# Queries and keys loaded by head and transposed block by block on VectorE, in a fused attention and two-stage MoE kernel

## The chip, the cores and the metric

The kernel runs on one core of a Trainium2 chip. The metric is the device time of one execution in microseconds (us), as the median of several runs. A core has five instruction streams that run side by side and meet only at semaphores: PE (TensorE, matrix multiply and transpose), DVE (VectorE), ACT (ScalarE), POOL (GpSimd) and SP (SyncE, which here issues every DMA transfer).

## What is computed

Four batches of four heads go through a linear attention whose feature map is the outer product of two 8-wide projections; the result, 4352 tokens of 128 values, goes through a normalised gated layer and then through a soft mixture of 8 experts. Everything is float32.

```python
# q, k, v: (4, 4, 1088, 32), S1, S2: (8, 32)
def phi(x):
    a = np.einsum('rd,bhsd->bhsr', S1, x)
    b = np.einsum('rd,bhsd->bhsr', S2, x)
    return np.einsum('bhsi,bhsj->bhsij', a, b).reshape(*x.shape[:-1], r * r)
q_p, k_p = (phi(q), phi(k))
kv = np.einsum('bhsf,bhsd->bhfd', k_p, v)
z = np.sum(k_p, axis=2)
num = np.einsum('bhsf,bhfd->bhsd', q_p, kv)
den = np.einsum('bhsf,bhf->bhs', q_p, z)[..., None] + 1e-06
attn = num / den
# x = attn as 4352 rows of H * D = 128
rms = np.sqrt(np.mean(x * x, axis=-1, keepdims=True) + 1e-06)
xn = x / rms * rms_g
y = (silu(xn @ w_gate) * (xn @ w_val)) @ w_out      # w_gate, w_val: (128, 1536)
# soft mixture on y: logits = y @ phi (32 slots), softmax over the tokens, the 8 experts
# on their slots (two matrices each), softmax over the slots, and back to the tokens
```

## The kernel before, in words

Each engine's program is written out by hand, in order, and every hand-over is a semaphore with a fixed count. Nothing is scheduled by a tool, so the order in the code is the order on the engine.

A batch has 1088 tokens: eight tiles of 128 tokens (TM = 8) and a remainder of 64 (SR). The queries are worked in nine blocks, two of 512 tokens (HT = 4 tiles) for each batch (blocks 0 to 7) and one of 256 tokens (block 8) with the four remainders.

**The front** prepares the keys and the first query block. It runs over 12 groups G, three for each batch (NG), of three tiles each (G3). SP loads keys, values and queries into tiles that have tokens on the partitions. For batches 0 and 1 DVE brings the keys of a group from the order (head, tile, d) to (tile, head, d) in `k_tok` (L760); for batches 2 and 3 POOL does it in one copy of a whole batch (L376). PE transposes the three tiles (`key_transposes`, L1022), ACT copies the result from PSUM to `kT` (L519), PE projects it (`key_projections`), ACT copies one of the two projections (L525), DVE multiplies the two to the features `kp` (L768), and PE adds features times values up to the moments (`moments`). DVE copies the moments out once for each batch (L750, `head_moments`). Between the groups stand the steps of query block 0: `queries_by_token` (DVE L619), `queries_T` (PE L882, ACT L437), `projections`, `features` (DVE L628, L630), `features_T` (PE L902, ACT L445), `attention` (PE, then DVE L640 to L650), `squares` (ACT L451), `mean_square` (DVE L657), the inverse root on POOL (L382), `normalised` (DVE L666), `normalised_T` (PE L925, ACT L455) and `split_x` (DVE L672, L674). The three weight matrices of the gated layer are split in a high and a low part on the way: ACT writes the high parts (L506), POOL the low ones (`wgl` L379, `wvl` L384, `wol` L386), in its order wgl, inverse root of block 0, wvl, wol.

**The blocks.** `whole_block` runs over 12 chunks c of 128 hidden columns. In each chunk PE does three matmuls for the gate, three for the value (`gate_value`) and three for the output of three chunks earlier (`output`); ACT takes silu of the gate (L476) and the high part of the hidden values (L484), DVE multiplies gate and value (L695) and forms the low part (L701). The attention of block j + 1 is spread over block j: in the kernel before, `queries_T` at c = 0, `projections` at c = 1, `features_T` at c = 2, `attention` at c = 4, `normalised_T` at c = 7. Every fp32 matmul and transpose is one row in the trace that ends at a line of a helper: L859 is the matmul helper.

**The end** computes the softmaxes and the experts, and SP stores the tokens.

## Time and profile before

| | before |
|---|---|
| median of 3 runs | 333.32 us (331.68 to 333.97) |
| span of the profiled execution | 332.9 us |
| PE busy | 304.8 us (92%) |
| DVE busy | 226.0 us (68%) |
| ACT busy | 176.2 us (53%) |
| POOL busy | 33.3 us (10%) |
| share of PE in the chain that ended last | 83% |

The profiled execution is 0.4 us shorter than the median of the runs; all start times below are counted from its own start. The span falls in three stretches: the front from 0 to 46.7 us, when the first matmul of block 0 starts; the nine blocks from there to about 300 us; and the end. A line of the timeline gives an operation's start, its length, engine and line of the kernel, what it writes and reads, how many instructions it groups, and in square brackets how long the engine had been idle before it and whose signal ended that. "area" is one of the large shared buffers, "bank" is PSUM. The chain of waits is read backwards from the last instruction and names what each piece waited for last.

### The profile page before, as it was taken

The page shows a single profiled execution, that of the slowest core. Times are in us where ns is not written, and L with a number is a line of the kernel's source. Part 1 is how long each engine was busy: PE and PEld are TensorE (multiplying, and loading weights), DVE is VectorE, ACT ScalarE, POOL GpSimd, SP SyncE. Part 2 cuts the span into 40 slices and gives each one's busy share as a digit, 9 for nine tenths or more (in the row PEclk, how much of TensorE's full clock was granted, in tenths as well). Part 3 has the DMA queues.
Part 4 walks back from the last instruction along what each step waited for, and adds up shares of the span by engine and source line. Part 5 has one row for each costly group of instructions (what it writes and reads, how often), then busy time and mean ns, then how long its engine had stood idle before and what let it go on. Part 6 is the DMA issues. An engine that isn't in the chain of part 4 may idle for free.

```text
span 332.9 us, 6852 instructions
## 1 busy us (share of the span) xinstructions
PE 304.8 (92%) x2596; PEld 245.2 (74%) x2596; DVE 226.0 (68%) x442; ACT 176.2 (53%) x333; POOL 33.3 (10%) x51
## 2 busy tenths in 40 slices
PE   1997539999999999999999999999999999997993
PEld 1786437878888878878888787888878778895472
DVE  4657765686858667775866777676677667974364
ACT  2657206555556654665665465566645656555410
POOL 1116470010001001100100110010001001001000
PEclk9999778999999999999999999999999999999997
DMA  6995019100100000059500000000000000000008
GB/s 185 301 346 139 3 36 417 53 0 2 63 2 1 0 3 2 0 156 290 121 0 0 0 0 0 0 0 0 0 0 1 0 2 0 3 0 3 2 22 248
DMA packets 25654, 19.97 MB, mean 60 GB/s; under 512 B 4129, under 2 KB 24353, under 8 KB 25633
## 3 DMA queue, kind: packets, MB, share of 16 engines
q1 hardware_dynamic: 25632, 19.68, 20.1%
q8 instruction: 14, 0.23, 0.3%
q14 instruction: 8, 0.06, 0.1%
HBM read 17.45 MB, written 2.23 MB: 59 GB/s over the span
## 4 chain that ended last, share of the span: by engine, by line
PE 83%; DVE 9%; ACT 3%; issue 2%; DMA 1%; SPq 0%; POOL 0%; DVEq 0%; ACTq 0%
PE bank L859 74%; PE bank L902 2%; DVE y_nat L850 2%; PE bank L1022 2%; DVE xh L672 2%; PE bank L945 1%; DVE area L666 1%; PE bank L925 1%; DMA area<-in_k 1%; PE bank L882 1%; DVE hl L701 1%; PE bank L1128 1%; DVE hid L695 1%; ACT woh L506 0%; DVE ssq L657 0%
## 5 line engine op out<-in xcount | busy, mean ns | idle before, releaser
L695 DVE TENSOR_TENSOR hid<-bank,silu 128x512 f32<-128x512 f32 (+1 forms) x108 | 71.3, 661 | 72.8 <-PE bank L859 58.9
L476 ACT ACTIVATE silu<-bank 128x512 f32<-128x512 f32 (+1 forms) x108 | 61.8, 572 | 81.7 <-PE bank L859 80.1
L701 DVE TENSOR_TENSOR hl<-hid,hh 128x512 fp32r<-128x512 f32 (+1 forms) x108 | 70.6, 654 | 0.1
L484 ACT ACTIVATE hh<-hid 128x512 fp32r<-128x512 f32 (+1 forms) x108 | 64.7, 599 | 0.9 <-PE bank L859 0.7
L859 PE MATMUL bank<-xh,wgh 128*128 128x512 f32 (+1 forms) x117 | 47.8, 408 | 6.2 <-DVE xl L674 5.9
L859 PE MATMUL bank<-xh,wgl 128*128 128x512 f32 (+1 forms) x117 | 44.9, 384 | 0.0
L859 PE MATMUL bank<-xl,wgh 128*128 128x512 f32 (+1 forms) x117 | 44.9, 384 | 0.0
L859 PE MATMUL bank<-hh,woh 128*128 128x512 f32 (+1 forms) x108 | 43.8, 405 | 0.4 <-DVE hl L701 0.4
L859 PE MATMUL bank<-xh,wvl 128*128 128x512 f32 (+1 forms) x108 | 41.6, 385 | 0.0
L859 PE MATMUL bank<-xh,wvh 128*128 128x512 f32 (+1 forms) x108 | 41.5, 385 | 0.0
L859 PE MATMUL bank<-xl,wvh 128*128 128x512 f32 (+1 forms) x108 | 41.2, 382 | 0.0
L859 PE MATMUL bank<-hh,wol 128*128 128x512 f32 (+1 forms) x108 | 41.1, 380 | 0.0
L859 PE MATMUL bank<-hl,woh 128*128 128x512 f32 (+1 forms) x108 | 40.9, 378 | 0.0
L859 PEld LDWEIGHTS bank<-xh,wgh 128*128 128x128 f32 x117 | 22.4, 192 | 10.5 <-issue 6.0
L401 POOL TENSOR_TENSOR rstd<-msq,mhalf 128x4 f32<-128x4 f32 (+1 forms) x8 | 7.8, 970 | 189.2 <-DVE msq L659 189.2
L859 PEld LDWEIGHTS bank<-xh,wgl 128*128 128x128 f32 x117 | 22.4, 191 | 4.6
L859 PEld LDWEIGHTS bank<-xl,wgh 128*128 128x128 f32 x117 | 22.5, 192 | 3.6
L859 PEld LDWEIGHTS bank<-xl,wvh 128*128 128x128 f32 x108 | 20.6, 190 | 4.2
L859 PEld LDWEIGHTS bank<-xh,wvl 128*128 128x128 f32 x108 | 20.6, 190 | 4.2
L859 PEld LDWEIGHTS bank<-hh,woh 128*128 128x128 f32 x108 | 20.3, 188 | 4.6 <-DVE hl L701 0.6
L859 PEld LDWEIGHTS bank<-xh,wvh 128*128 128x128 f32 x108 | 20.6, 190 | 4.0
L859 PEld LDWEIGHTS bank<-hh,wol 128*128 128x128 f32 x108 | 20.3, 188 | 4.1
(151 smaller groups left out, 372.4 us busy)
## 6 DMA issues: line engine op xcount, KB each, us to landing
area<-in_moe_w SPq DMA_DIRECT2D x1, 4096.0 KB, 12.7
area<-in_moe_w SPq DMA_DIRECT2D x8, 512.0 KB, 7.3
area<-in_k SPq DMA_DIRECT2D x4, 512.0 KB, 6.2
y_nat<-in_v SPq DMA_DIRECT2D x4, 512.0 KB, 6.4
q_in<-in_q SPq DMA_DIRECT2D x4, 512.0 KB, 4.3
out<-y_nat SPq DMA_DIRECT2D x8, 256.0 KB, 2.9
area<-in_moe_w_gate SPq DMA_DIRECT2D x1, 768.0 KB, 8.2
area<-in_moe_w_val SPq DMA_DIRECT2D x1, 768.0 KB, 8.8
```

The costliest lines, as they stand in the source:

```text
L401: pool.tensor_tensor(rstd[:, 0:nt], msq[:, 0:nt], mhalf[:, 0:nt], ALU.pow).then_inc(s_rstd_ready, 1)
L476: act.activation(silu[n][:, 0:w], gate_b[n][:, 0:w], ACT.Silu).then_inc(s_silu_ready, 1)
L484: act.activation(hh[m % NH][:, 0:w], hid[m % 2][:, 0:w], ACT.Copy).then_inc(s_hh_ready, 1)
L666: dve.tensor_tensor(x_n[:, 0:nt, :], x_at[:, 0:nt, :], rstd[:, 0:nt].unsqueeze(2).to_broadcast([P, nt, P]), ALU.mult).then_inc(s_xn_ready, 1)
L672: dve.tensor_copy(xh[n][:, 0:w], xT_raw[:, 0:w]).then_inc(s_xh_ready, 1)
L695: dve.tensor_tensor(hid[n][:, 0:w], val_b[n][:, 0:w], silu[n][:, 0:w], ALU.mult).then_inc(s_hid_ready, 1)
L701: dve.tensor_tensor(hl[m % NH][:, 0:w], hid[m % 2][:, 0:w], hh[m % NH][:, 0:w].bitcast(F32), ALU.subtract).then_inc(s_hl_ready, 1)
L850: dve.tensor_tensor(o_sb[:, HT * j:HT * j + nt, :], bank[2 + n % 6][:, 0:nt * P].rearrange("p (t d) -> p t d", d=P), crec[:, HT * j:HT * j ...
L859: return pe.matmul(o, l, r, start=start, stop=stop)
L882: ins = pe.transpose(bank_a[:, t * P:(t + 1) * P], tile, ident[:, :])
L902: ins = pe.transpose((bank_a, bank_c)[hp][:, t * P:(t + 1) * P], qp[:, t, hp * P:(hp + 1) * P], ident[:, :])
L1022: ins = pe.transpose(kT_b[:, t * P:(t + 1) * P], k_tok[G // NG % 2][:, G3 * (G % NG) + t, :, :].rearrange("p h d -> p (h d)"), ident[:, :])
```

## The change

Queries and keys are loaded with the 32 partitions of a head holding 32 runs of consecutive tokens of that head (`"h (u n) d -> h u (n d)"`), so that a key transfer of 8 tiles has one run of 4 KB for each of the 128 partitions, where it had four of 1 KB; the remainder has one run of 256 B on 128 partitions, where it had four of 128 B on 64. The queries are loaded by half batch, with one run of 2 KB on each partition and a semaphore for each half. DVE then transposes 32x32 blocks straight from the loaded tile to `kT` and `qT`. This is the transposed layout that the projections read, since head h occupies the 32 partitions from 32h on both sides. The values' tile (partition p holds tokens 8p to 8p + 7) and the tokens of a key tile stay matched. The tokens of a query block are now 512 consecutive ones, and the store of the output follows that.

What falls away: on PE the 36 key transposes and the 34 query transposes; on ACT the 12 copies to `kT` and the 9 to `qT`; on DVE the six copies L760 and the four L619; on POOL the two copies L376. What comes: on DVE one transpose for each key group (4 x 96 columns, or 4 x 64 and another of 2 x 32 for the third group of a batch) and one for each query block (4 x 128 columns; 256 for block 8). `kT` now holds a whole batch, twice, so that DVE runs four groups ahead: groups 0 to 3 stand ahead of the loop, group G + 4 behind the features of group G.

Of the diff, the loads, ACT's copy to `kT`, the two new functions of DVE and their calls in the front, the wait that `features_T` takes over on PE, and the store (in this order):

```diff
-        k_in = [area1[:, n * KW:(n + 1) * KW].rearrange("p (h t d) -> p h t d", h=H, t=TK) for n in range(B)]
-        k_tok = [area1[:, (B + n) * KW:(B + n + 1) * KW].rearrange("p (t h d) -> p t h d", h=H, t=TK) for n in range(2)]
-        kT = [area1[:, (B + 2) * KW + n * G3 * P:(B + 2) * KW + (n + 1) * G3 * P] for n in range(2)]
+        KB_MAIN, KB_REM = TM * P // D, SR // D
+        KC = (KB_MAIN + KB_REM) * D
+        k_in = [area1[:, n * KC:(n + 1) * KC] for n in range(B)]
+        kT = [area1[:, B * KC + n * TK * P:B * KC + (n + 1) * TK * P] for n in range(2)]
...
-        q_in = sb("q_in", [P, H, TM, D])
-        q_rem = sb("q_rem", [P, 2, H, D])
-        q_tok = sb("q_tok", [P, TM, H * D])
+        q_in = sb("q_in", [P, 2, W])
+        q_rem = sb("q_rem", [P, B, SR // D, D])
...
+            def load_queries(b, half):
+                sp.dma_start(q_in[:, half, :],
+                             q[b, :, half * W:(half + 1) * W, :].rearrange("h (u k) d -> h u (k d)", u=D))\
+                    .then_inc(s_q_loaded[half], 16)
+
             for b in range(B):
-                for src, dst, loaded in ((k, k_in[b], k_loaded[b]), (v, v_in[b], v_loaded[b])):
-                    sp.dma_start(dst[:, :, 0:TM, :],
-                                 src[b, :, 0:TM * P, :].rearrange("h (p t) d -> p h t d", t=TM)).then_inc(loaded, 16)
-                    sp.dma_start(dst[0:SR, :, TM, :],
-                                 src[b, :, TM * P:S, :].rearrange("h p d -> p h d")).then_inc(loaded, 16)
+                sp.dma_start(k_in[b][:, 0:KB_MAIN * D],
+                             k[b, :, 0:TM * P, :].rearrange("h (u n) d -> h u (n d)", u=D)).then_inc(k_loaded[b], 16)
+                sp.dma_start(k_in[b][:, KB_MAIN * D:KC],
+                             k[b, :, TM * P:S, :].rearrange("h (u n) d -> h u (n d)", u=D)).then_inc(k_loaded[b], 16)
...
+            sp.wait_ge(s_qT_ready, 1)
+            load_queries(1, 0)
             sp.wait_ge(s_kv_ready, B)
             sp.dma_start(w1_sb, w1.rearrange("e d f -> d e f")).then_inc(s_w1_loaded, 16)
+            for n in range(3, 2 * B):
+                sp.wait_ge(s_qT_ready, n - 1)
+                load_queries(n // 2, n % 2)
...
-                if G < B * NG:
-                    act.wait_ge(s_kT_ps, G + 1)
-                    if later(G - 1):
-                        act.wait_ge(s_kab_ps, G - 1)
-                    act.activation(kT[G % 2], kT_b[:, 0:G3 * P], ACT.Copy).then_inc(s_kT_ready, 1)
...
+            def queries_T(jn, half, b):
+                if isinstance(jn, int) and jn == NB:
+                    dve.wait_ge(s_qrem_loaded, 16 * B)
+                    src = q_rem[:, :, :, :]
+                    dst = qT[:, 0:B * SR].rearrange("p (b u r) -> p b r u", b=B, r=SR // D)
+                else:
+                    dve.wait_ge(s_q_loaded[half], b * 16 + 16)
+                    src = q_in[:, half, :].rearrange("p (i t d) -> p i t d", i=P // D, t=HT)
+                    dst = qT.rearrange("p (t u i) -> p i t u", t=HT, i=P // D)
+                if later(jn):
+                    dve.wait_ge(s_ab_ps, jn)
+                dve.transpose(dst, src).then_inc(s_qT_ready, 1)
+
+            def keys_T(G):
+                b, g = G // NG, G % NG
+                if g == 0:
+                    dve.wait_ge(k_loaded[b], 32)
+                if later(G + 1 - 2 * NG):
+                    dve.wait_ge(s_kab_ps, G + 1 - 2 * NG)
+                t0, t1 = G3 * g, min(G3 * g + G3, TM)
+                src = k_in[b][:, 0:KB_MAIN * D].rearrange("p (i t d) -> p i t d", i=P // D, t=TM)
+                dst = kT[b % 2][:, 0:TM * P].rearrange("p (t u i) -> p i t u", t=TM, i=P // D)
+                ins = dve.transpose(dst[:, :, t0:t1, :], src[:, :, t0:t1, :])
+                if g == NG - 1:
+                    ins = dve.transpose(kT[b % 2][:, TM * P:TM * P + SR].rearrange("p (u r) -> p r u", r=KB_REM),
+                                        k_in[b][:, KB_MAIN * D:KC].rearrange("p (r d) -> p r d", r=KB_REM))
+                ins.then_inc(s_kT_ready, 1)
...
+            for G in range(4):
+                keys_T(G)
             for G in range(B * NG):
...
                 if G % NG == 1 and G > NG:
                     head_moments(G // NG - 1)
+                if G + 4 < B * NG:
+                    keys_T(G + 4)
                 if G == 2:
-                    queries_by_token(0, 0)
+                    queries_T(0, 0, 0)
...
+                if later(jn):
+                    pe.wait_ge(s_xT_ready, jn)
...
-                    rows = out[b * S:b * S + TM * P, :].rearrange("(p t) d -> p t d", t=TM)
-                    sp.dma_start(rows[:, t0:t0 + HT, :], o_sb[:, j * HT:(j + 1) * HT, :]).then_inc(s_out_stored, 16)
+                    rows = out[b * S + t0 * P:b * S + (t0 + HT) * P, :].rearrange("(p t) d -> p t d", t=HT)
+                    sp.dma_start(rows, o_sb[:, j * HT:(j + 1) * HT, :]).then_inc(s_out_stored, 16)
```

The first place is PE inside the blocks, at the change from chunk c = 0 to c = 1. Before, these are the rows there; `hh` and `wo` belong to `output`, `xh` and `w` to `gate_value`, and `q_tok` is the query tile in token order.

```order
L859 MATMUL bank<-hh,woh 128x512 [waits hl_ready]
L859 MATMUL bank<-hl,woh 128x512
L859 MATMUL bank<-hh,wol 128x512
L877 REGISTER_ALU
L882 MATMUL bank<-ident,q_tok 128x128 [waits xT_ready,qtok_ready]
L882 MATMUL bank<-ident,q_tok 128x128 x3
L962 REGISTER_ALU
L859 MATMUL bank<-xh,wgh 128x512 [waits hid_ready]
```

And now, where L858 is the matmul helper of the changed kernel:

```order
L858 MATMUL bank<-hh,wol 128x512
L950 REGISTER_ALU
L858 MATMUL bank<-xh,wgh 128x512 [waits hid_ready]
L858 MATMUL bank<-xl,wgh 128x512
L858 MATMUL bank<-xh,wgl 128x512
L858 MATMUL bank<-xh,wvh 128x512
L858 MATMUL bank<-xl,wvh 128x512
L858 MATMUL bank<-xh,wvl 128x512
L872 REGISTER_ALU
L874 REGISTER_ALU [waits qT_ready]
```

The four transposes have gone from between the output of one chunk and the gate of the next; the projections one chunk later still wait for `qT_ready`, which is now DVE's signal and not ACT's.

The second place is DVE in the front, from the features of group 0 on. Before (L768 features of a key group, L619 queries to token order):

```order
L760 COPY area<-area 128x384 [waits k_loaded1]
L760 COPY area<-area 128x384 x2
L768 TENSOR_TENSOR area<-bank,logit 128x768 [waits kb_ready]
L768 TENSOR_TENSOR comb<-bank,logit 128x768 [waits kb_ready]
L768 TENSOR_TENSOR logit<-bank,logit 128x768 [waits kb_ready]
L619 COPY q_tok<-q_in 128x1024 [waits q_loaded]
L768 TENSOR_TENSOR area<-bank,logit 128x768 [waits kb_ready,kmom_done]
L768 TENSOR_TENSOR comb<-bank,logit 128x768 [waits kb_ready,kmom_done]
```

And now (L618 and L620 transpose keys, L607 queries, L765 is the features' line):

```order
L618 STREAM_TRANSPOSE area<-area 128x4x96 [waits k_loaded1]
L765 TENSOR_TENSOR area<-bank,logit 128x768 [waits kb_ready]
L618 STREAM_TRANSPOSE area<-area 128x4x96
L765 TENSOR_TENSOR comb<-bank,logit 128x768 [waits kb_ready]
L618 STREAM_TRANSPOSE area<-area 128x4x64
L620 STREAM_TRANSPOSE area<-area 128x2x32
L765 TENSOR_TENSOR logit<-bank,logit 128x768 [waits kb_ready]
L618 STREAM_TRANSPOSE area<-area 128x4x96 [waits kab_ps,k_loaded2]
L607 STREAM_TRANSPOSE area<-q_in 128x4x128 [waits q_loaded0]
L765 TENSOR_TENSOR area<-bank,logit 128x768 [waits kb_ready,kmom_done]
L618 STREAM_TRANSPOSE area<-area 128x4x96 [waits kab_ps]
```

Three copies in a row behind the arrival of batch 1 have become one transpose, and behind every group's features up to group 7 stands another one; the keys of batches 2 and 3, which POOL had, are now in DVE's row too.

## Rows read from the trace of the kernel before

**Rows 1.** The page, its head and part 1: busy time of each engine.
```profile
span 332.9 us, 6852 instructions
PE 304.8 (92%) x2596; PEld 245.2 (74%) x2596; DVE 226.0 (68%) x442; ACT 176.2 (53%) x333; POOL 33.3 (10%) x51
```
**Rows 2.** Busy time by window: length, then busy us of each engine, clock, DMA.
```profile
74.33:103.96 29.63, 29.63 (x209) 23.95 (x209) 20.65 (x37) 16.86 (x30) 1.01 (x1) 1.00 0.06 19
103.96:133.59 29.63, 29.63 (x210) 23.96 (x209) 20.80 (x39) 17.37 (x32) 1.41 (x2) 1.00 0.01 2
10.19:30.34 20.15, 18.36 (x387) 15.62 (x386) 14.42 (x29) 12.98 (x28) 5.75 (x3) 1.00 1.01 293
```
**Rows 3.** The chain that ended last, one block: start, length, what.
```profile
103.96 10.99 PE bank L859 x48
114.95 0.44 PE bank L882 x4
115.39 4.97 PE bank L859 x34
```
**Rows 4.** Query transposes on PE, grouped by form.
```profile
L882 PE MATMUL bank<-ident,q_tok 128*128 128x128 f32 x32 | 4.8, 273 | 0.0
```
**Rows 5.** What PE waited for, whole span: us, times, longest.
```profile
PE bank L859 <- DVE xl L674: 5.9, 1, 5.9
PE bank L925 <- DVE area L666: 4.3, 2, 3.8
```
**Rows 6.** Timeline of DVE in the front.
```profile
10.19 1.47 DVE L760 COPY area<-area 128x384 f32<-128x384 f32 x3 [2.78 <-DMA area<-in_k]
26.14 0.96 DVE L768 TENSOR_TENSOR comb<-bank,logit 128x768 f32<-128x768 f32 x1 [3.14 <-ACT logit L525]
...
28.11 0.25 DVE L643 RECIPROCAL rden<-den 128x16 f32<-128x16 f32 x1
...
30.34 0.69 DVE L657 TENSOR_REDUCE ssq<-area 128x4 f32<-128x512 f32 x1 [0.32 <-ACT area L451]
...
32.36 3.90 DVE L666 TENSOR_TENSOR area<-area,rstd 128x512 f32<-128x512 f32 x1 [0.27 <-POOL rstd L382]
...
40.64 5.22 DVE L672 CAST xh<-area 128x512 fp32r<-128x512 f32 x1 [1.01 <-ACT area L455]
```
**Rows 7.** Timeline of POOL in the front.
```profile
15.65 1.15 POOL L376 COPY area<-area 128x1152 f32<-128x1152 f32 x1 [13.30 <-DMA area<-in_k]
19.36 1.15 POOL L376 COPY area<-area 128x1152 f32<-128x1152 f32 x1 [2.56 <-DMA area<-in_k]
...
26.86 3.46 POOL L379 TENSOR_TENSOR wgl<-area,wgh 128x1536 fp32r<-128x1536 f32 x1 [6.35 <-ACT wgh L506]
31.30 1.02 POOL L382 TENSOR_TENSOR rstd<-msq,mhalf 128x4 f32<-128x4 f32 x1 [0.99 <-DVE msq L659]
32.30 3.42 POOL L384 TENSOR_TENSOR wvl<-area,wvh 128x1536 fp32r<-128x1536 f32 x1
```
**Rows 8.** Timeline of ACT in the front.
```profile
23.70 0.84 ACT L506 ACTIVATE wgh<-area 128x768 fp32r<-128x768 f32 x1 [2.14 <-DMA area<-in_moe_w_gate]
...
30.70 0.85 ACT L506 ACTIVATE wvh<-area 128x768 fp32r<-128x768 f32 x1
```
**Rows 9.** DVE instructions that price a transpose, grouped by form: busy us, mean ns.
```profile
L657 DVE TENSOR_REDUCE ssq<-area 128x4 f32<-128x512 f32 x8 | 5.4, 679 | 0.3 <-ACT area L451 0.3
L760 DVE COPY area<-area 128x384 f32<-128x384 f32 x6 | 2.9, 546 | 4.6 <-DMA area<-in_k 4.6
L619 DVE COPY q_tok<-q_in 128x1024 f32<-128x1024 f32 x4 | 2.7, 685 | 0.0
L724 DVE TENSOR_REDUCE cmax_a<-logit 128x32 f32<-128x896 f32 x1 | 1.8, 1792 | 0.0
L836 DVE TENSOR_REDUCE csum<-comb 128x34 f32<-128x1088 f32 x1 | 1.3, 1276 | 0.0
L797 DVE TENSOR_REDUCE cmax<-logit 128x32 f32<-128x192 f32 x1 | 0.5, 502 | 0.0
```
**Rows 10.** DMA packets in the windows 6 to 10 us and 52 to 58 us.
```profile
DMA packets 1697, 1.21 MB, mean 303 GB/s; under 512 B 576, under 2 KB 1697, under 8 KB 1697
DMA packets 609, 2.49 MB, mean 416 GB/s; under 512 B 0, under 2 KB 0, under 8 KB 609
```
**Rows 11.** Timeline of DVE in a block, around c = 0.
```profile
114.37 0.69 DVE L695 TENSOR_TENSOR hid<-bank,silu 128x512 f32<-128x512 f32 x1 [0.77 <-PE bank L859]
114.98 0.68 DVE L701 TENSOR_TENSOR hl<-hid,hh 128x512 fp32r<-128x512 f32 x1
116.89 0.69 DVE L695 TENSOR_TENSOR hid<-bank,silu 128x512 f32<-128x512 f32 x1 [1.23 <-PE bank L859]
```

More of the change, by code:

```diff
@@ L170, in fused_attention_moe @@
         s_wo_loaded = sem("wo_loaded")
-        s_q_loaded = sem("q_loaded")
+        s_q_loaded = [sem(f"q_loaded{n}") for n in range(2)]
         s_qrem_loaded = sem("qrem_loaded")
@@ L370, in _ @@
             pool.memset(kv[:, :, :, :], 0.0).then_inc(s_kvpads_ready, 1)
-            pool.wait_ge(s_kpads_ready, B)
-            for b in range(2, B):
-                pool.wait_ge(k_loaded[b], 32)
-                pool.wait_ge(s_kT_ps, (b - 1) * NG)
-                pool.tensor_copy(k_tok[b % 2], k_in[b].rearrange("p h t d -> p t h d")).then_inc(s_ktok23_ready, 1)
             pool.wait_ge(s_wg_hi, 2)
@@ L492, in whole_block @@
                     step(j, c)
-                    if c == 0 and not last:
-                        queries_T(j + 1)
                     if c == 2 and not last:
@@ L591, in _ @@
         def _(dve):
-            for n in range(B):
-                dve.memset(k_in[n][SR:P, :, TM, :], 0.0).then_inc(s_kpads_ready, 1)
+            for n in range(2):
+                dve.memset(kT[n][:, TM * P + SR:TK * P], 0.0).then_inc(s_kTpads_ready, 1)
             for n in range(B):
@@ L706, in whole_block @@
                 for c in range(-LAG if first else 0, C):
-                    if c == 0 and odd and nb is not None:
-                        queries_by_token(j + 1, nb)
+                    if c == 0 and not last:
+                        queries_T(j + 1, odd ^ 1, nb)
                     step(j, c)
@@ L752, in head_moments @@
                 ins.then_inc(s_kv_ready, 1)
-            dve.wait_ge(s_kpads_ready, B)
-            for b in range(2):
-                dve.wait_ge(k_loaded[b], 32)
-                for g in range(NG):
-                    tiles = slice(g * G3, (g + 1) * G3)
-                    dve.tensor_copy(k_tok[b][:, tiles], k_in[b].rearrange("p h t d -> p t h d")[:, tiles])\
-                        .then_inc(s_ktok01_ready, 1)
+            for G in range(4):
+                keys_T(G)
             for G in range(B * NG):
@@ L783, in _ @@
             head_moments(B - 1)
-            whole_block(0, 0, first=True)
+            whole_block(0, 0, 0, first=True)
             with dve.Fori(1, B) as b:
@@ L869, in _ @@
             pe.wait_ge(s_sblk_ready, H)
-            def queries_T(jn, half, b):
-                if isinstance(jn, int) and jn == NB:
-                    pe.wait_ge(s_qrem_loaded, 16 * B)
-                    tiles = [q_rem[:, n, :, :].rearrange("p h d -> p (h d)") for n in range(2)]
-                else:
-                    pe.wait_ge(s_qtok_ready, b + 1)
-                    tiles = [q_tok[:, HT * half + t, :] for t in range(HT)]
-                if later(jn):
-                    pe.wait_ge(s_xT_ready, jn)
-                for t, tile in enumerate(tiles):
-                    ins = pe.transpose(bank_a[:, t * P:(t + 1) * P], tile, ident[:, :])
-                ins.then_inc(s_qT_ps, 1)
             def projections(jn):
```

66 lines of the change are left out of this document (16 added, 50 removed).

## The prediction

> **What bounds the kernel now.** The page comes first: PE is busy for 304.8 of 332.9 us, DVE for 226.0 [rows 1]. Such shares are means over stages, so the windows come next. A whole block takes 29.63 us, and in it PE is busy for 29.63 us, DVE for 20.7 (twice the same to 0.2 us) [rows 2]. The chain of waits of a block is made of PE alone; what is taken off PE there comes off the time, and DVE has 8.9 us to spare. One piece of that chain is the query transposes, 0.44 us [rows 3].
>
> The front is another matter. The table of PE's waits has 5.9 us in front of the first matmul of block 0 and 4.3 for L666 [rows 5]. The timelines show why. DVE's L666 takes 3.90 us, where L657 on as many elements takes 0.69, and it starts 0.06 us after POOL's wvl of 3.42 us; L672 takes 5.22 us behind wol in the same way [rows 6, 7]. So from L657 at 30.34 on, the front is one chain: mean square, inverse root to 32.32, wvl and L666 to 36.3, the last two groups, wol and L672, first matmul at 46.7. It starts later or earlier as L657 does. Ahead of L657 DVE had to wait: of 20.15 us from the arrival of key batch 1 to L657 it is busy for 14.42, so idle for 5.7 [rows 2]. The longest wait, 3.14 us ahead of 26.14, is for ACT, which itself waited for w_gate until 23.70 and so copied features_T late [rows 6, 8].
>
> **Blocks: query transposes leave PE.** They are issued 8 times with four tiles, once in the front and for blocks 1 to 7 [rows 4], and with two for block 8. In the chain of a block the four cost 0.44 us. 7 x 0.44 = 3.1, and half of 0.44 for block 8: **-3.3 us**. All other PE work stays. DVE loses L619 of 685 ns every second block and gets a transpose of 512 columns in every block. Whatever this costs between 0.68 and 1.09 us (below), it stands at c = 0 ahead of L695, where DVE sits idle for 0.77 us waiting for PE in the chunks around [rows 11]; what is over delays L695 by 0.3 us at most, and idle time of the same size stands ahead of the next one. DVE's total goes to some 21.5 of 29.2 us. Projections wait one chunk later, 2 us on. If that cover were gone, PE would wait with L695 and the whole 1.09 us would show eight times, once in each block from 0 to 7. ACT's 0.6 us copy was off the chain: nothing. The queries' loads are issued a block or two ahead and w2's after them, over 100 us before their use: nothing. The store has as many runs of 512 B as before: nothing.
>
> **Front: what the transfers give.** From 6 to 10 us the loads run at 303 GB/s in runs of 1 KB and below; w1 with runs of 4 KB runs at 416 [rows 10]. 524 KB of a key batch then take 1.26 instead of 1.73 us, 0.45 less, and the remainder half as many packets. The arrival of batch 1 (10.19) moves up by two of these, 1.0 us with the smaller remainder, to 9.2; w_gate has four of them (1.8) and the queries in 2 KB runs (estimated 0.3) ahead of it, so it is there at 21.6. Bounds: nothing, and these.
>
> **Front: what DVE gets.** No row shows a transpose on DVE, nor a write with a step. Lower bound, one element per cycle: L760 has 546 ns for 384 elements and L657 679 for 512; L657 and L836 make 1.04 ns for one more element and 0.15 us at the start. Upper bound: L724 and L797 read with each element 128 bytes on, 1792 ns for 896 and 502 for 192, so 1.83 ns each [rows 9]. The transpose writes with a step of 16 bytes. From L657 back to the arrival of batch 1 there are six transposes of 384, three of 256 with one of 64, and one of 512:
> - low price: 6 x 0.55 + 3 x (0.41 + 0.21) + 0.68 = 5.8 us
> - high price: 6 x 0.85 + 3 x (0.62 + 0.27) + 1.09 = 8.9 us
>
> Off go three L760 (1.47, rows 6) and L619 (0.68): 14.42 - 2.15 = 12.3 us stay. At the high price DVE is busy for 21.2 us from 9.2 on; that fills its former idle time, and some 0.4 us of waits remain: L657 at 30.8, **+0.4 us**. At the low price it is 18.1 us and about 1.3 of waits (features_T through PE and ACT stay on the way to group 7): 28.6, -1.7 us. I take the high price: the write's step puts no two elements next to each other, and of the rows only L724 and L797 do that. **A wait moves to DVE.** The keys of batches 2 and 3, which POOL fetched at 15.65 and 19.36 [rows 7], are now waited for by DVE itself, and behind that instruction stand the query transpose, the features of group 3 and all that follows. DVE comes there after three features (2.9 us) and three groups of transposes: at the high price 9.2 + 2.9 + 2.6 = 14.7, at the low one 13.8, against an arrival at some 14.1 (three key batches and the queries earlier by 1.6). So 0.3 us at the low price, nothing at the high one; batch 3 is in by 17.5, before DVE is through group 5.
>
> ACT's twelve copies and PE's key transposes were hidden beside DVE and w_gate and give nothing by themselves; what PE no longer does only shortens the way from kT to kb. Behind L657 all stays: the high part of w_val (ready at 31.55, inverse root at 32.32 [rows 7, 8]) is still first, so wvl still catches L666.
>
> The notes speak against this edit: the Trainium skill, "SBUF — State Buffer", on the port swizzle (its box on cachelines), says that each access which moves on to another 16-byte line pays a penalty; by that the high price holds, +0.4 us here, and the reads of L724 and L797 agree, while no row shows it for a write.
>
> **Sum.** 332.9 - 3.3 + 0.4 = 330.0 us of span; the median of the runs is 0.4 above the profiled execution, so **330.4 us** (329.8 to 331.4, the upper end with none of the transfers' gain: batch 1 at 10.2 gives L657 at 31.8).
>
> **Rivals.**
> - *Transposes at the low price.* For it speaks that DVE's contiguous copies and reductions keep to a cycle each, and writes need not behave like reads. -3.3 - 1.7: 328.3 us (327.7 to 330.0, the upper end with w_gate as late as before and group 7 again behind it). Chance 0.33. The Trainium skill, "VectorE: DVE Perf Modes", section "The three transpose paths", has 311 ns for 128x128 in bf16; an estimate from this page's figure is the low price and this time. No row here has a transpose on DVE to hold against it.
> - *DVE's transposes are held up by POOL like L666.* wgl (3.46 us) follows the high part of w_gate and would lie on the keys of group 10 or 11: +2.5 us on the forecast, 332.9. Against it: L666 and L672 read SBUF through what POOL uses, but L643, one input in SBUF, took 0.25 us in the middle of wgl's 3.46 and so was not held up [rows 6, 7]. Chance 0.05.
> - *A transpose of 4-byte data takes several passes.* This is the rival on the other side. 6 x 384 + 3 x 320 + 512 = 3776 elements lie ahead of L657, and thirteen starts of 0.15 us, 1.95 us. To lose 1% (3.3 us) over no change the front must give 6.6 us more, L657 at 37.0 instead of 30.3: 27.8 us of work from 9.2 on, of which 12.3 stay, 13.5 go to the elements: 3.6 ns each, twice the high price. At four cycles (4.2 ns) it is +8.9 - 3.3, 338.9 us. Between 1.83 and 3.6 ns it ends within 1%. Chance 0.07 beyond 3.6, 0.08 between 2.3 and 3.6 (332 to 336.6).
> - *The inverse root gets in ahead of wvl.* If the high part of w_val came over 0.8 us later, L666 would run in 0.7 and save 3.2 us: 327.2. ACT has less to do, so this moves away. 0.02.
>
> **How the numbers follow.** Forecast 0.45, low price 0.33, POOL 0.05, dearer 0.08 and 0.07, inverse root 0.02. About 1% is what a measurement of this kernel can tell from no change, 330.0 us downwards and 336.7 upwards. Faster: 0.33 + 0.02 and a third of the forecast's 0.45, since 330.4 stands so near 330.0: 0.50. Slower: 0.07. Same: 0.43. The range 327.6 to 333.6 takes in both prices with and without the transfers' gain and POOL's hold, and leaves out the dearer transposes and the inverse root, 0.17.
>
> **What would show it.** Right: blocks of 29.2 us, with PE busy throughout and no new wait on DVE L697 or qT; keys' transposes of 0.85 us for 384 columns; key batch 1 in by 9.2 and w_gate by 21.6 us; no wait of DVE above 1 us between groups 3 and 8; first matmul of block 0 at about 47.1 us. Wrong: 0.55 us per transpose, first matmul at 45; or a transpose far above 1 us, with PE and ACT idle in the front; or a block of 29.6, which would mean that the transposes had been hidden on PE after all.

## The result and the profile after

| | before | after |
|---|---|---|
| median of the runs (range) | 333.64 us (331.68 to 334.18) | 353.72 us (352.26 to 354.22) |
| span of the profiled execution | 332.9 us | 351.4 us |
| first matmul of block 0 | 46.73 us | 69.45 us |
| a whole block | 29.63 us | 29.17 us |
| key batch 1 / w_gate in use | 10.19 / 23.70 us | 20.10 / 45.86 us |

The change makes the kernel slower: ratio 1.0594, interval 1.0551 to 1.0637. The first matmul of block 0 comes 22.7 us later, and what follows it takes 281.95 us instead of 286.17, 4.2 us less. The blocks gave what was forecast, and the front lost five times as much.

The page of the kernel after: busy time, then the granted clock, the share of the 16 DMA engines that is busy and what they move, in 40 slices of 8.8 us.

```profile
PE 299.0 (85%) x2526; PEld 243.1 (69%) x2526; DVE 235.8 (67%) x455; ACT 166.0 (47%) x312; POOL 31.3 (9%) x49
...
PE   0141583499999999999999999999999999998993
...
PEclk9996567689999999999999999999999999999999
DMA  4444840084000000000000794000000000000008
GB/s 89 134 137 133 246 132 17 2 343 167 0 0 32 0 3 30 2 1 4 26 0 0 138 271 98 0 0 0 0 0 0 2 0 3 0 2 2 0 8 248
```

PE is fully at work from the ninth slice on; up to then it mostly waits, and the DMA engines are busy for four tenths at 89 to 137 GB/s (in the fifth slice for eight tenths, at 246), where the front before had 303 [rows 10]. The waits of the kernel after, over the whole span (waiting engine and line, who ends the wait, total, times, longest):

```profile
POOL wgl L373 <- ACT wgh L494: 46.3, 1, 46.3
...
DVE area L618 <- DMA area<-in_k: 25.0, 4, 8.2
...
ACT area L516 <- DMA y_nat<-in_v: 11.6, 1, 11.6
```

DVE waited for keys four times, 25.0 us. The chain of waits goes through the last key batch: the second of its two loads is issued at 29.97 us, and the batch is there 12.45 us later.

```profile
29.97 12.45 DMA area<-in_k
```

In DVE's timeline these waits stand in brackets, and the rest of the front follows (start, length, line):

```profile
12.10 2.01 DVE L618 STREAM_TRANSPOSE area<-area 128x384 f32<-128x384 f32 x3 [8.12 <-DMA area<-in_k]
...
20.10 0.85 DVE L618 STREAM_TRANSPOSE area<-area 128x384 f32<-128x384 f32 x1 [5.93 <-DMA area<-in_k]
...
33.10 0.85 DVE L618 STREAM_TRANSPOSE area<-area 128x384 f32<-128x384 f32 x1 [8.16 <-DMA area<-in_k]
33.80 1.05 DVE L607 STREAM_TRANSPOSE area<-q_in 128x512 f32<-128x512 f32 x1
...
42.45 0.86 DVE L618 STREAM_TRANSPOSE area<-area 128x384 f32<-128x384 f32 x1 [2.83 <-DMA area<-in_k]
...
53.29 0.69 DVE L659 TENSOR_REDUCE ssq<-area 128x4 f32<-128x512 f32 x1 [0.60 <-ACT area L441]
...
55.31 3.90 DVE L668 TENSOR_TENSOR area<-area,rstd 128x512 f32<-128x512 f32 x1 [0.27 <-POOL rstd L376]
...
63.59 4.98 DVE L674 CAST xh<-area 128x512 fp32r<-128x512 f32 x1 [1.01 <-ACT area L445]
```

Key batch 3 is in use at 42.45 us, where POOL had it at 19.36 [rows 7], 23.1 us late; the mean square (L659, before L657 at 30.34 [rows 6]) starts 22.95 us late. Behind it all is as it was, 3.90 us beside wvl included. A whole block, by windows (length, busy us of PE, PEld, DVE, ACT, POOL, clock, DMA share, GB/s), against [rows 2]:

```profile
95.82:125.00 29.18, 29.18 (x205) 23.56 (x205) 20.92 (x37) 16.28 (x29) 1.01 (x1) 1.00 0.03 10
125.00:154.17 29.17, 29.17 (x206) 23.57 (x205) 21.64 (x40) 16.80 (x31) 1.41 (x2) 1.00 0.03 10
```

And DVE's transposes by form (busy us, mean ns):

```profile
L607 DVE STREAM_TRANSPOSE area<-q_in 128x512 f32<-128x512 f32 x8 | 8.8, 1100 | 0.0
...
L618 DVE STREAM_TRANSPOSE area<-area 128x384 f32<-128x384 f32 x8 | 6.7, 856 | 25.0 <-DMA area<-in_k 25.0
...
L618 DVE STREAM_TRANSPOSE area<-area 128x256 f32<-128x256 f32 x4 | 2.6, 642 | 0.1
...
L607 DVE STREAM_TRANSPOSE area<-q_rem 128x256 f32<-128x256 f32 x1 | 0.4, 439 | 0.0
```

The last two lines have 256 columns each, and only the first of them costs the high price. It writes with a step of 16 bytes; the transpose of the query remainders (`q_rem`, two tokens of a head to a partition) writes with a step of 8 bytes.

So blocks, transposes and order came out as forecast, and the transfers did not. What slows them? Theory A: the number of engines that carry a DMA load is the largest one, up to 16, that divides the sizes of the outermost parts of both its patterns. The keys' source now begins with the 4 heads, so each load of keys and queries runs on 4 engines; before, it began with 128 token groups. The Trainium skill, "DMA: Bandwidth & Descriptors", section "Why a DMA increments its semaphore by 16 and not by 1", states this rule, with the lowest-numbered engines taken, so that such loads also share the same ones. The trace agrees: from 10 to 12 us, where key batch 1 is under way with the end of the values, the engines' share is 0.28. Rivals: DVE's new place in the chain (it now waits for the keys itself), or something in the loads' size, number or order of addresses.

### The profile page after: what moved, and what is told of

Its sections match the earlier page's. It is cut to its first block, busy times and chain, and to the rows that moved or that the text cites. A ratio compares the mean times of both kernels' runs of the same rounds, so it can differ in the third digit from the quotient of the medians.

```text
span 351.4 us, 6670 instructions
## 1 busy us (share of the span) xinstructions
PE 299.0 (85%) x2526; PEld 243.1 (69%) x2526; DVE 235.8 (67%) x455; ACT 166.0 (47%) x312; POOL 31.3 (9%) x49
## 4 chain that ended last, share of the span: by engine, by line
PE 75%; DVE 8%; SPq 8%; DMA 4%; ACT 2%; issue 1%; POOL 0%; DVEq 0%; ACTq 0%
PE bank L858 68%; SPq L316 4%; DMA area<-in_k 4%; PE bank L890 2%; SPq L312 2%; DVE y_nat L849 2%; DVE xh L674 1%; PE bank L933 1%; DVE area L668 1%; PE bank L913 1%; SPq L310 1%; DVE hl L703 1%; PE bank L1100 1%; DVE hid L697 1%; SPq L305 1%
## 5 line engine op out<-in xcount | busy, mean ns | idle before, releaser
L858 PE MATMUL bank<-xh,wgh 128*128 128x512 f32 (+1 forms) x117 | 46.9, 400 | 5.3 <-DVE xl L676 5.0
L858 PE MATMUL bank<-xh,wgl 128*128 128x512 f32 (+1 forms) x117 | 45.0, 384 | 0.0
L858 PE MATMUL bank<-xl,wgh 128*128 128x512 f32 (+1 forms) x117 | 44.6, 382 | 0.0
L858 PE MATMUL bank<-hh,woh 128*128 128x512 f32 (+1 forms) x108 | 43.8, 405 | 0.4 <-DVE hl L703 0.4
L858 PE MATMUL bank<-xh,wvh 128*128 128x512 f32 (+1 forms) x108 | 41.4, 384 | 0.0
L858 PE MATMUL bank<-xh,wvl 128*128 128x512 f32 (+1 forms) x108 | 41.4, 383 | 0.0
L858 PE MATMUL bank<-hh,wol 128*128 128x512 f32 (+1 forms) x108 | 41.1, 380 | 0.0
L858 PE MATMUL bank<-xl,wvh 128*128 128x512 f32 (+1 forms) x108 | 41.0, 380 | 0.0
L858 PE MATMUL bank<-hl,woh 128*128 128x512 f32 (+1 forms) x108 | 40.9, 379 | 0.0
L858 PE MATMUL bank<-s_blk,area 128*64 128x64 f32 x280 | 15.2, 264 | 25.6 <-DVE area L618 10.0
L858 PEld LDWEIGHTS bank<-s_blk,area 128*64 128x64 f32 x280 | 12.7, 171 | 29.6 <-issue 21.4
L858 PEld LDWEIGHTS bank<-xh,wgh 128*128 128x128 f32 x117 | 22.3, 190 | 9.7 <-issue 5.1
L618 DVE STREAM_TRANSPOSE area<-area 128x384 f32<-128x384 f32 (+1 forms) x12 | 9.1, 785 | 25.1 <-DMA area<-in_k 25.0
L858 PEld LDWEIGHTS bank<-xh,wgl 128*128 128x128 f32 x117 | 22.3, 190 | 4.5
L858 PEld LDWEIGHTS bank<-xl,wgh 128*128 128x128 f32 x117 | 22.4, 191 | 3.9
L858 PEld LDWEIGHTS bank<-xl,wvh 128*128 128x128 f32 x108 | 20.6, 190 | 4.2
L858 PEld LDWEIGHTS bank<-hh,woh 128*128 128x128 f32 x108 | 20.3, 188 | 4.6 <-DVE hl L703 0.6
```

Source lines behind the costliest of these rows:

```text
L618: ins = dve.transpose(dst[:, :, t0:t1, :], src[:, :, t0:t1, :])
L858: return pe.matmul(o, l, r, start=start, stop=stop)
```

## The experiments

**The loads alone, in the kernel before.** Key loads as in the change, all else as before:

```diff
-  sp.dma_start(k_in[b][:, :, 0:TM, :], k[b, :, 0:TM*P, :].rearrange("h (p t) d -> p h t d", t=TM))
+  sp.dma_start(k_flat[:, 0:TM*P],      k[b, :, 0:TM*P, :].rearrange("h (u n) d -> h u (n d)", u=D))
```

> The kernel before with one part of the change alone: the keys (main part and remainder) are loaded in the changed form, head by head with 32 runs of 4 KB each; all else is as before, so keys and values no longer match by token and the output differs. Theory A (the key and query loads whose source pattern starts with the 4 heads run on a quarter of the DMA engines: in the changed kernel's trace the DMA share stands at 0.2 to 0.3 and 98 GB/s while they run, some 5.2 us for 524 KB): key batches arrive at about 12, 20, 28 and 37 us, w_gate after 40, first matmul of block 0 near 63, time near 350 us, DMA share near a quarter for long stretches. Theory B (DVE's transposes or the new order of the front are the cause): 333 to 335 us, since neither is in this kernel.

354.46 us, ratio 1.0614 (1.0575 to 1.0653): as slow as the whole change, with PE and ACT still transposing keys and queries. DVE's first two key copies waited 8.22 and 7.27 us for keys, w_gate was used at 41.94, and the first matmul of block 0 came at 66.53, a little after the 63 expected. The loss is there without anything that DVE does in the change. (The two kernels are not the same sum: this one has neither the blocks' gain nor the slow query loads.)

**The other way round.** The kernel after, with the main key loads, and then the query loads too, in the form of before (same bytes and work, other places):

> The changed kernel with the main part of the keys loaded in the old form (128 partitions first, four runs of 1 KB each); the key remainder, the queries, the transposes and the order stay as changed. The transposes then work on keys in another token order, so the output differs, not the work. Theory A: the keys cost 1.7 us each again, only the two loads for query block 0 and 1 are still slow (5.2 us together, 3.6 more than before) and push batches 2 and 3 and w_gate back; first matmul near 52 us, time 334 us. Theory B: no change from the changed kernel, 353 us. Theory C (the remainder's small runs of 256 B stop the queue, on whose issue SP stands for up to 7.5 us): no change either, 350 to 353 us.

> As the run before, and the queries' loads too in a form with 128 partitions first (runs of 512 B); token order and so output differ. This leaves of the change what DVE, PE, ACT and POOL do. Theory A: arrivals as in the kernel before, first matmul at 48 to 49 us (the transposes at 0.85 us for 384 columns, as priced), blocks of 29.2 us: 330 to 331 us. Theories B and C: near 350 us.

Keys alone: 337.68 us, 1.0085 (1.0057 to 1.0112). Keys and queries: 332.31 us, 0.9946 (0.9923 to 0.9969), key batches used at 6.13, 10.23 and 16.02 us, w_gate at 23.38, first matmul at 47.80. The keys' loads carry 16 us of the loss and the queries' 5.4. Both kernels are slower than was expected for them: 337.68 against 334 (first matmul 53.12 against 52), and 332.31 against 330 to 331, part of it because the kernel before took 334.04 beside them and not 333.32. DVE of the second kernel, its key waits and the mean square:

```profile
6.13 2.02 DVE L618 STREAM_TRANSPOSE area<-area 128x384 f32<-128x384 f32 x3 [2.16 <-DMA area<-in_k]
...
10.23 0.86 DVE L618 STREAM_TRANSPOSE area<-area 128x384 f32<-128x384 f32 x1 [2.02 <-DMA area<-in_k]
...
31.42 0.67 DVE L659 TENSOR_REDUCE ssq<-area 128x4 f32<-128x512 f32 x1
```

**Cut into four, cut into two.** The same runs and addresses as after, as one load per head (keys and queries), and as one load per two heads (keys):

```diff
-  sp.dma_start(k_in[b][:, 0:1024], k[b, :, 0:1024, :].rearrange("h (u n) d -> h u (n d)", u=D))
+  for h in range(H):        # e4
+      sp.dma_start(k_in[b][h*D:(h+1)*D, 0:1024], k[b, h, 0:1024, :].rearrange("(u n) d -> u (n d)", u=D))
+  for x in range(2):        # e8
+      sp.dma_start(k_in[b][x*64:(x+1)*64, 0:1024], k[b, 2*x:2*x+2, 0:1024, :].rearrange("h (u n) d -> h u (n d)", u=D))
```

> The changed kernel, whole, with the same runs from the same addresses to the same places, but each key and query load issued as four, one for each head, so that 32 runs and not 4 heads come first in each. Theory A: every piece is spread over all engines; key batch 1 in by 9 to 10 us, w_gate by 22 to 25 (SP has 17 more issues of about 0.5 us), first matmul at 47 to 50 us, time 329 to 332 us. Theory D (runs of 4 KB from this layout are slow in themselves, by their length or addresses): still 350 us. Theory C: still near 350 us, since the remainder is unchanged.

> The kernel after, with each of the four main key loads cut into two, one for two heads each; same bytes, runs and addresses, nothing left out. Theory A (the outermost part of a load's pattern sets how many of the 16 engines carry it, and always the first ones): a load for two heads is carried by two engines, and both halves by the same two, so the cut makes it worse. The first two engines then carry 2.1 MB of keys between them, in the kernel after four did; with the other loads that is 1.5 MB to an engine instead of 1.0 MB, and at the 25 GB/s per engine of the kernel after (about 100 GB/s on four) the last weight comes some 20 us later: 370 to 378 us. Rival B (each load has its own engines or its own rate, so more loads run side by side, as the cut into four loads gained 18 us): between the kernel after (353.7 us) and the cut into four (335.4 us), about 345 us.

One load of four heads 353.72 us, two loads 373.54 (ratio 1.1186, from two runs), four loads 335.39 (1.0040). Cutting once makes it 20 us worse, cutting again 38 us better, of which the queries, cut only in the second kernel, can hold some 5 (above). An effect of the loads' size, number or addresses alone would not turn round like this, and theory A had the 373.5 in its 370 to 378. The windows show the engines counted out. First the kernel after, then the one with head pairs, both where hardly anything but keys is under way:

```profile
10.00:12.00 2.00, 0.00 (x0) 0.00 (x0) 0.00 (x0) 0.00 (x0) 0.00 (x0) 1.00 0.28 84
```

```profile
10.00:12.00 2.00, 0.00 (x0) 0.00 (x0) 0.00 (x0) 0.00 (x0) 0.00 (x0) 1.00 0.13 51
12.00:14.00 2.00, 0.00 (x0) 0.00 (x0) 0.00 (x0) 0.00 (x0) 0.00 (x0) 1.00 0.13 51
14.00:16.00 2.00, 0.00 (x0) 0.00 (x0) 0.00 (x0) 0.00 (x0) 0.00 (x0) 1.00 0.13 49
```

0.13 of 16 is 2 engines, 0.28 is 4 and a little. 51 GB/s over two is 25 GB/s each, about what 416 GB/s over 16 make [rows 10]; in the kernel after it is 19 GB/s each in this window. So with pairs each engine runs near its full rate, and there are too few of them.

By-head loads do not get all of it back: 335.39 us where 329 to 332 were expected, key batch 1 at 11.12 us and w_gate at 28.33. The number of loads is part of it: SP issues w_gate at 21.12 us, where before it did so at 15.48. But the DMA engines were not idle either. These are the windows from 6 to 14 us of the kernel before and of this one (the last two columns are the DMA share and GB/s; the share adds up the time of the packets, so it can pass 1):

```profile
6.00:14.00 8.00, 6.08 (x72) 4.53 (x72) 5.02 (x9) 4.10 (x9) 0.00 (x0) 1.00 1.12 310
```

```profile
6.00:14.00 8.00, 2.43 (x40) 2.30 (x42) 4.88 (x8) 1.55 (x3) 0.00 (x0) 1.00 1.04 250
```

At nearly the same share they moved a fifth less. Each of these loads goes to 32 partitions only; e9 and e10 below show the same with values.

**Keys of a whole batch in one load.** 34 tokens of one head to a partition are one run of 4352 B, and 128 of them the whole batch:

```diff
-  k[b, :, 0:1024, :].rearrange("h (u n) d -> h u (n d)", u=D)      # and one for the remainder
+  k[b].rearrange("h (u n) d -> (h u) (n d)", u=D)                  # e5; e6: "h (u n) d -> h u (n d)"
-  dst = kT[...].rearrange("p (t u i) -> p i t u", ...)
+  dst = kT[...].rearrange("p (t i u) -> p i t u", ...)             # dense writes
```

> The kernel after, with the loads of the front in a form whose outermost part is long, so that on theory A they are spread over 16 engines: a key batch is one load of 128 rows of 4352 B (34 tokens of one head to a partition, remainder included), the values follow in six loads of 32 partitions (same tokens, 1 KB and 128 B runs), the first 512 queries in four loads by head, the second 512 behind the weights. The key transposes also write densely now (each 32 outputs side by side), while the query transpose still writes with its 16-byte step. All work is done, nothing is left out. Theory A (few engines per load were the whole loss): key batch 1 in by 9, no wait of VectorE above 2 us in the front, w_gate in by 23, blocks of 29.17 us, and a time below the kernel before. On the price of the transposes: if the 16-byte step of the write is what made them 0.85 us for 384 columns, they take 0.55 us now beside 1.09 us for the 512 queries, the mean square starts at about 29 us, and the time is 328.5 to 329.5 us; if it is the transpose itself, they stay at 0.85 us, the mean square starts at 30 to 31 us and the time is 330 us. Rival (the transfers are slow because of short runs or the number of bytes): batch 1 after 12 us, time above 335 us.

> e5 with one thing changed: the source of each key load is written as 4 heads x 32 rows x 4352 B in place of 128 rows x 4352 B. Same bytes, same addresses, same 128 runs, same number of loads. Theory A in its strict form (the outermost part as written decides how many engines a load gets): key batches come as late as in the kernel after (batch 1 after 12 us, w_gate after 30 us), time 345 to 352 us. If neighbouring dimensions are merged before the engines are chosen, there is no difference to e5. Rival (something in the order of addresses): also no difference to e5, since the addresses are the same.

e5 333.86 us (0.9995, 0.9966 to 1.0024), e6 334.62 (1.0009, 0.9974 to 1.0043): no difference between them. With 34 of 34 tokens the heads follow each other without a gap, so 4 x 32 rows are 128 rows, and the way it is written does not matter. In the change, 1024 of 1088 tokens leave a gap between heads, and the 4 stays outermost. Theory A in its strict form (345 to 352 us expected for e6) is ruled out; it holds for the pattern after such merging.

e5 missed its 328.5 to 329.5 us, though. The price part came true: the dense key transposes take 565 ns for 384 columns, while the query transpose, still with the 16-byte step, keeps its price in the same kernel:

```profile
L621 DVE STREAM_TRANSPOSE area<-area 128x384 f32<-128x384 f32 x8 | 4.4, 565 | 7.7 <-DMA area<-in_k 7.7
...
L610 DVE STREAM_TRANSPOSE area<-q_in 128x512 f32<-128x512 f32 x1 | 1.1, 1056 | 0.0
```

But DVE still waited 7.7 us for keys. Two kernels took this apart: values loaded in two loads as before (e9), and by head to all 128 partitions (e10).

> e5 with the values loaded as in the kernel before, in two loads of 128 and 64 partitions for a batch instead of six of 32 partitions. The rows of values then belong to other tokens than the keys they are paired with; the work is the same. In e5 the 16 engines were busy all the time from 6 to 18 us and yet moved only 241 GB/s, against 316 in the query-part-alone kernel. If the value loads of 32 partitions are what is slow: above 290 GB/s from 6 to 14 us, key batch 1 in by 9.5 instead of 11.35 us, batch 2 by 14 instead of 17.4, w_gate by 23, and 329 to 330 us. If it is the key load with rows of 4352 B: rates and arrivals as in e5, 333 to 334 us.

> e5 with the main part of the values in four loads by head, each to all 128 partitions, instead of four by groups of 32 partitions; the key transposes write with their 16-byte step again, since the tokens of a partition are others. Nothing is left out. If a load to 32 partitions is what is slow, the transfers are those of e9: key batch 1 by 9.5 us, w_gate by 23 us; VectorE has 0.28 us more for each key transpose, 2 us in all before the mean square, of which the waits that fall away give back as much: 330 to 331 us. If the number of loads is what is slow (SyncE issues 32 of them at 0.46 us before w_gate), w_gate is as late as in e5 and the time is 334 to 335 us.

The window 6 to 14 us of e5, e9 and e10, in this order (last two columns: DMA share, GB/s):

```profile
6.00:14.00 8.00, 2.46 (x41) 2.33 (x43) 3.84 (x8) 1.56 (x3) 0.00 (x0) 1.00 1.10 244
```

```profile
6.00:14.00 8.00, 3.96 (x69) 3.83 (x70) 5.02 (x11) 2.86 (x5) 0.00 (x0) 1.00 1.06 322
```

```profile
6.00:14.00 8.00, 3.49 (x60) 3.36 (x62) 5.20 (x11) 2.55 (x5) 0.00 (x0) 1.00 0.74 223
```

e9: 329.58 us, 0.9864 (0.9825 to 0.9904), within its forecast; key batch 1 used at 9.87 us, w_gate at 21.50, first matmul at 45.33. (It pairs keys with values of other tokens, so it shows a time and is no kernel to use.) e9 also has fewer loads than e5; e10, with as many as e5, separates the two. For each full share of the 16 engines e5 moved 222 GB/s (244 over 1.10), e9 304 and e10 301. So the value loads of 32 partitions are what slowed e5: all engines busy, each a quarter slower. The Trainium skill, "SBUF — State Buffer", section "Door 1: The DMA port swizzle", has a transfer's rate go by the SBUF ports that its partitions reach; 244 against 322 GB/s agrees in direction, and no run here gives a rate for such loads by themselves. e10: 333.43 us, 0.9989 (0.9955 to 1.0024), not the 330 to 331 expected: key batch 1 at 10.07 us, but the engines only 0.74 busy and w_gate not before 25.48. For w_gate SP is the limit: four value loads take it 2.5 us to issue, 0.62 us each, in every batch, and it issues w_gate at 20.65 us, where e9 does so at 11.51:

```profile
12.13 2.48 SPq L312 DMA_DIRECT2D y_nat<-in_v  x4
```

Both causes exist, one in each kernel, and I had not expected the second to remain. It is the smaller part, though. The mean square starts 3.3 us later than in e9: DVE is busy 2.0 us longer from key batch 1 on (19.55 against 17.53 us), since its transposes cost 865 ns again with the 16-byte step, and it waits 1.0 us more for ACT, which waits for w_gate.

**The query half alone.** The kernel before, with queries transposed by DVE and keys untouched (the first 512 queries in four loads by head):

> The kernel before with the query half of the change alone: queries transposed by VectorE, no PE transposes and ScalarE copies of queries; keys and values are loaded and transposed as before. The first 512 queries come in four loads by head, the second 512 behind the weights. If the gain of the change sits wholly in the blocks: 8 blocks 0.46 us shorter, -3.7 us, and in the front the query transpose of 1.09 us takes the place of a copy of 0.68 us, +0.4 us: 3.3 us under the kernel before, 330.5 us, blocks of 29.17 us, first matmul of block 0 within 0.7 us of 46.7. If the keys' half also carries some of the block gain, the blocks stay above 29.17 us.

330.53 us, 0.9901 (0.9863 to 0.9939), as expected for the time. Blocks of 29.17 us: the chain of this kernel has L856 after the transposes at 98.35 and the same at 127.52.

```profile
97.91 0.44 PE bank L911 x4
98.35 15.94 PE bank L856 x82
...
127.09 0.44 PE bank L911 x4
127.52 2.52 PE bank L856 x11
```

All the block gain is the query half's. The profiled execution was the quickest of the eight (326.78 us): the first matmul came at 43.30 us, not within 0.7 of 46.7, and 2.05 us of that are the high part of x, which took 3.17 us in it instead of 5.22. It ended at 42.43, with POOL's product wol (to 42.14); in the kernel before it ended at 45.86, after POOL's memset behind wol (to 45.35). What the slower executions do is not traced.

**POOL beside DVE.** The length of these instructions beside POOL's led to two kernels that let POOL's products wait until DVE is through:

```diff
+  pool.wait_ge(s_xn_ready, 1)     # e11 and e12, ahead of wvl
   pool.wait_ge(s_wv_hi, 2)
...
+  pool.wait_ge(s_xl_ready, 1)     # e12, ahead of wol
   pool.wait_ge(s_wo_hi, 2)
```

> The query-part-alone kernel with one more wait: POOL computes the low part of w_val (wvl) behind VectorE's normalisation of block 0 (the instruction that takes 3.90 us beside wvl, 0.7 us alone on as many elements) instead of just ahead of it. Nothing is left out. If wvl beside it is what makes it 3.90 us: it takes 0.7 us, all that follows moves up by 3.2 us, wvl is done by 36 us and still in time for its first matmul; 327.3 us. The low part of w_out still lies on the high part of x (5.2 us). If its length has another cause: 3.90 us as before, and 330.5 us or, with wvl later, up to 331.

> The kernel of e11 with a second wait of the same kind: the low part of w_out (wol) behind VectorE's high and low part of x. If wol beside it is what makes the high part 5.22 us, it takes 0.7 us and the first matmul of block 0 comes 4.5 us earlier still, at about 38 us; 322.8 to 324 us. If PE then waits in block 0 for wol, up to 1 us of that is lost. If the length has another cause: as e11.

e11: 326.77 us, 0.9784 (0.9755 to 0.9813). e12: 319.66 us, 0.9573 (0.9545 to 0.9602), the quickest kernel here, 4.3% under the one before. DVE and POOL of e12 (before: 3.90 and 5.22 us for the two [rows 6]):

```profile
32.20 0.69 DVE L665 TENSOR_TENSOR area<-area,rstd 128x512 f32<-128x512 f32 x1 [0.27 <-POOL rstd L382]
...
36.48 0.43 DVE L671 CAST xh<-area 128x512 fp32r<-128x512 f32 x1 [1.01 <-ACT area L452]
```

```profile
32.97 3.46 POOL L385 TENSOR_TENSOR wvl<-area,wvh 128x1536 fp32r<-128x1536 f32 x1 [0.81 <-DVE area L665]
...
37.71 3.53 POOL L388 TENSOR_TENSOR wol<-area,woh 128x1536 fp32r<-128x1536 f32 x1 [1.28 <-DVE xl L673]
```

With nothing of POOL beside it the normalisation takes 0.69 us and the cast 0.43. In e11, where wvl ends at 36.4 and wol follows at once, the cast took 5.66 us, past wol and past POOL's memset behind it. The Trainium skill, "SBUF — State Buffer", section "Who interferes with whom", says that a port pair shared by VectorE and GpSimd is locked for a whole instruction; these rows agree for both forms. e12 gained 7.1 us over e11, where 4.5 at most were expected for the cast. The rest is TensorE's clock. PE in e11 and then e12, its first matmuls of block 0 and, below, the window from there on:

```profile
42.95 0.77 PE L857 MATMUL bank<-xh,wgh 128*128 128x512 f32 x1 [6.11 <-DVE xl L672]
43.52 0.63 PE L857 MATMUL bank<-xl,wgh 128*128 128x512 f32 x1
```

```profile
42.95:55.00 12.05, 12.04 (x59) 9.57 (x60) 8.54 (x15) 5.62 (x11) 1.47 (x6) 0.87 0.86 335
```

```profile
37.77 0.47 PE L858 MATMUL bank<-xh,wgh 128*128 128x512 f32 x1 [0.87 <-DVE xl L673]
38.08 0.40 PE L858 MATMUL bank<-xl,wgh 128*128 128x512 f32 x1
```

```profile
37.77:50.00 12.23, 12.22 (x70) 9.96 (x71) 9.94 (x17) 6.55 (x12) 8.40 (x12) 1.00 0.88 335
```

e12's 322.8 to 324 us was missed by 3 us on the good side. After a wait of 6.1 us PE starts at 0.63 us a matmul, and the mean clock of the next 12 us is 0.87 (the lower of the two levels, 1.2 GHz, for a part of it); after a wait of 0.87 us it starts at 0.40, at 2.4 GHz throughout. 13% of 12 us is 1.6 us. Of the 6.6 us between the two spans, 5.2 are the earlier first matmul and 1.4 lie behind it.

## Why the prediction was wrong

- **Blocks, -3.3 us: right.** 29.17 us forecast as 29.2, PE busy throughout, no new wait. It is 0.46 instead of 0.44 us a block, and with seven blocks of four transposes and one of two that makes 3.4 us. Behind the first matmul 4.2 us are gone in all. The other 0.8 are TensorE's clock and no merit of the edit: PE waited 5.0 us ahead of its first matmul instead of 5.9, and in the 12 us behind it the granted clock was 0.82 instead of 0.75 (before, then after; the clock is the third number from the end):

```profile
46.73:58.73 12.00, 12.00 (x55) 9.40 (x56) 5.88 (x12) 5.66 (x10) 1.47 (x6) 0.75 0.86 331
```

```profile
69.45:81.45 12.00, 12.00 (x56) 9.50 (x57) 7.91 (x15) 5.07 (x9) 1.77 (x7) 0.82 0.86 332
```

- **What the transfers give: this step failed.** It took the rate from the length of the runs (4 KB runs at 416 GB/s) and looked for no other property. w1's load, from whose rows it took the rate, has a source of 128 rows outermost; the new key loads have 4. Forecast: key batch 1 by 9.2 us, w_gate by 21.6. Measured: 20.10 and 45.86. The bounds were "nothing, and these", a gain in both cases, though ten loads ahead of w_gate were rewritten and no row of before showed a load of that form. By theory A and the forecast's own row: keys and queries ahead of w_gate are 2.7 MB, over four engines of 26 GB/s 26 us, instead of about 9 at the front's 303 GB/s: 17 us late (an estimate), of the 22.2 measured. That was to be had from the diff. The gain of 1.0 us for batch 1 was too high as well: in e9, with the keys in long runs over all engines, it is in use at 9.87, 0.3 us earlier than before.
- **What DVE gets: the price was right, its cause too.** High price 0.85 and 1.09 us, measured 856 and 1100 ns; e5 shows that it is the write's step, 565 ns without it, and e10, with the step again, 865. It is the step of 16 bytes and not any step: with 8 bytes 256 columns take 439 ns, as in e5 without a step (429), and with 16 bytes 642. The Trainium skill, "SBUF — State Buffer", on the port swizzle (its box on cachelines), which the prediction cited against the edit, asks for at least two accesses to each 16-byte line; it is borne out for this write. The 311 ns for 128x128 that the prediction set beside the low price, from the Trainium skill, "VectorE: DVE Perf Modes", make with a start of 0.15 us an estimate of 0.63 us for 384 columns, not the low price of 0.55.
- **The front without the transfers' gain: right.** For that case the prediction had the mean square at 31.8 and 331.4 us, 1.9 us under the 333.3 of the kernel before. With keys and queries loaded as before (e3) the mean square started at 31.42, the first matmul came 1.1 us later than before, and the median was 332.3 us, 1.7 under the 334.0 of the kernel before beside it. So without the failed step the change is worth 0.5%, and the forecast of 330.4 and the chance of 0.50 for faster by over 1% rested on a gain of the transfers that did not come.
- **Time outside the span: put at nothing.** The prediction carried the kernel before's distance of 0.4 us from span to median over to the changed kernel. Compared run by run, the time lies 1.8 us above the span in the kernel before (1.75 to 1.86) and in e1, and 2.4 in the kernel after (2.42 to 2.46); it is 2.35 or more in every kernel with the keys' transposes on DVE. These 0.6 us are lost outside the trace, and their cause is open.
- **Waits moved to DVE.** Named, with the query transpose and group 3 behind the key wait; priced at 0 to 0.3 us for batch 2 and nothing for batch 3, measured 8.16 and 2.83, since the arrival it was held against was wrong (the other 14.05 of the 25.0 us are batches 0 and 1, for which DVE waited before too, 4.6 us). With the arrivals of before (e3) the wait for batch 2 is 0.96 us and there is none for batch 3, so the place of the wait costs little.
- **Rivals.** Low price: ruled out by 856 ns. POOL holding up the transposes: not seen; the two beside wgl (48.66 to 52.13) took 0.67 us for 256 columns and 0.22 for 64, as the others. Several passes: ruled out. Inverse root ahead of wvl: not seen. What is missing among them is a loss in the transfers.

## What to carry to other kernels

When a load's pattern is rewritten, write down the size of its outermost part, after merging neighbours without a gap, on both sides: the number of DMA engines follows it, and longer runs do not make up for 4 of 16. In the profile this looks like a flat DMA share of 0.25 or 0.13 with queued loads; check the share, not only GB/s. And where two engines stretch each other's instructions, a wait that puts them in turn can be worth more than the work removed: the second wait of this kind (e12 over e11) and the clock it kept gave 7 us.

## What the hardware showed that was not expected

- A transpose of 4-byte data on DVE costs 1.47 ns per column of 128 partitions at 384 columns written densely (565 ns) and 2.2 with a 16-byte step (856 ns). A step of 8 bytes cost nothing more (439 ns for 256 columns, 429 without a step).
- Cutting a load into more loads can make it slower (two pairs of heads, 373.5 us) or faster (four heads, 335.4 us).
- SP's issue of a load takes some 0.4 to 0.46 us here at best and 0.62 for the value loads of e10, so some 30 loads can be a limit of their own (e10: DMA share 0.74).
- Loads to 32 partitions kept all engines busy and moved a fifth to a quarter less (e4 250 GB/s, e5 244, against 310 and 322).
- Beside POOL's float32 products a cast on DVE grew from 0.43 to 5.66 us, longer than the product beside it (3.43 us): it ended at 42.08, after the next POOL instruction (to 41.57), which seems to have held it too.
